# Moving operands of the f32r matmuls placed 192 bytes beyond a multiple of 256 bytes in each partition, their weights on a multiple

## What is computed

```python
# 1: attention, 8 heads of 64, window of n_local = 96 and n_global = 8 first keys
scores = q @ k.T / 8 - slope[h] * dist          # masked where not kept
a = softmax(scores); x = a @ v                  # x: (2, 768, 512)
# 2: gate from a causal convolution of 5 taps over x
gate = sigmoid(conv5(x)); x = (gate * (x @ w_val)) @ w_out1
# 3: the same form with 1024 hidden channels and a centred convolution of 3 taps
h = relu(x @ w_in); y = (h * sigmoid(conv3(h))) @ w_out2
```

## Time and profile before

| | us |
|---|---|
| median of 3 runs | 270.22 (269.54 to 270.37) |
| profiled execution | 269.72 |
| span of its trace | 267.9 |
| PE busy | 261.0 (97%) |
| weight loads (PEld) busy | 205.9 (77%) |
| DVE busy | 190.0 (71%) |
| ACT busy | 151.6 (57%) |
| POOL busy | 47.4 (18%) |

### The profile page before, as it was taken

The page is one execution under the profiler, slowest core; times in us unless marked ns, Lnnn a source line. Parts: engine busy times, 40 slices in busy tenths (PEclk is TensorE's granted clock), DMA queues, the critical chain, the costliest instruction groups (busy, mean ns, idle before and its releaser), DMA issues.

```text
span 267.9 us, 4415 instructions
## 1 busy us (share of the span) xinstructions
PE 261.0 (97%) x1526; PEld 205.9 (77%) x1526; DVE 190.0 (71%) x467; ACT 151.6 (57%) x346; POOL 47.4 (18%) x70
## 2 busy tenths in 40 slices
PE   8899999999999989999999999999999999999995
PEld 7444558788778878888888888888888888888883
DVE  0388479999889977998950897988409998991000
ACT  1051569889998767343554407965537649753100
POOL 1012056695387621200000000000000000000000
PEclk9999999999999999999999999999999999999999
DMA  6999807686897111000000000000000003004021
GB/s 199 355 377 315 289 7 208 203 259 191 240 262 232 45 43 42 4 1 0 2 0 0 0 2 0 1 0 0 2 0 0 0 2 132 24 0 159 0 100 57
DMA packets 20263, 25.16 MB, mean 94 GB/s; under 512 B 3728, under 2 KB 10384, under 8 KB 20112
## 3 DMA queue, kind: packets, MB, share of 16 engines
q1 hardware_dynamic: 19088, 23.86, 27.9%
q10 hardware_dynamic: 1152, 1.01, 1.1%
HBM read 21.52 MB, written 3.34 MB: 93 GB/s over the span
## 4 chain that ended last, share of the span: by engine, by line
PE 85%; DVE 6%; DMA 4%; ACT 3%; issue 1%; ACTq 1%
PE ps L559 21%; PE ps L561 20%; PE ps L560 20%; PE ps L455 8%; PE ps L530 6%; PE ps L515 5%; PE ps L502 5%; DMA win<-in_win 4%; DVE prob L949 2%; ACT prob L699 1%; DVE probT L956 1%; DVE total_eps L960 1%; DVE g L977 1%; DVE xT L972 0%; ACT probT L706 0%
## 5 line engine op out<-in xcount | busy, mean ns | idle before, releaser
L699 ACT ACTIVATE prob<-prob,low 128x256 f32<-128x256 f32 (+1 forms) x96 | 45.9, 482 | 6.6 <-DVE low L949 6.4
L977 DVE SCALAR_TENSOR_TENSOR g<-xT,cw,g 128x512 f32<-128x512 f32 x48 | 34.3, 779 | 1.6 <-ACT g L734 1.6
L805 ACT ACTIVATE h<-ps 128x512 f32<-128x512 f32 x24 | 14.0, 595 | 31.2 <-PE ps L561 31.2
L949 DVE CUSTOM_DVE_ANT_0 prob<-ps,bias 128x256 f32<-128x256 f32 x80 | 30.4, 408 | 1.7 <-PE ps L502 1.7
L455 PE MATMUL ps<-win,w1t 128*128 128x512 f32 x56 | 24.7, 596 | 1.0 <-DMA win<-in_win 1.0
L559 PE MATMUL ps<-gh,Wh 128*128 128x512 f32 x64 | 24.9, 389 | 0.0
L561 PE MATMUL ps<-gh,Wl 128*128 128x512 f32 x64 | 24.9, 389 | 0.0
L561 PE MATMUL ps<-hghA,w2l 128*128 128x512 f32 x64 | 24.9, 389 | 0.0
L560 PE MATMUL ps<-hglA,w2h 128*128 128x512 f32 x64 | 24.9, 389 | 0.0
L559 PE MATMUL ps<-hghA,w2h 128*128 128x512 f32 x64 | 24.9, 389 | 0.0
L560 PE MATMUL ps<-gl,Wh 128*128 128x512 f32 x64 | 24.9, 389 | 0.0
(11 more groups left out here) (101 smaller groups left out, 527.7 us busy)
## 6 DMA issues: line engine op xcount, KB each, us to landing
q_rows<-in_q SPq DMA_DIRECT2D x12, 256.0 KB, 4.8
kW<-in_k SPq DMA_DIRECT2D x12, 256.0 KB, 5.2
v_own<-in_v SPq DMA_DIRECT2D x12, 256.0 KB, 3.3
invT<-inv_turned SPq DMA_DIRECT2D x20, 128.0 KB, 3.4
out<-xT SPq DMA_DIRECT2D x5, 512.0 KB, 2.8
w<-in_w SPq DMA_DIRECT2D x8, 256.0 KB, 11.0
v_win<-in_v SPq DMA_DIRECT2D x10, 192.0 KB, 3.3
prob<-in_wval SPq DMA_DIRECT2D x1, 1024.0 KB, 9.6
```

Source lines behind the costliest of these rows:

```text
L699: act.activation(part, part, ACT.Exp, scale=-1.0, bias=low[:, t % 2, i:i + 1], accum_out=total[:, t % 2, i:i + 1]).then_inc(exp_done, 1)
L805: act.activation(h_cols(m, c), pieces(HB(m), c), ACT.Relu).then_inc(relu_done, 1)
L949: dve.tensor_tensor_reduce(prob[:, t % 2, i, cols], SC(f, e)[:, i % HH // 2, cols], table, -SCALE, 3.0e38, ALU.add, ALU.min, low[:, t % 2, ...
L977: dve.scalar_tensor_tensor(out=pieces(g[:, m, :], c), in0=x_cols(m, c, tap - PAD1), scalar=cw1[:, m, tap:tap + 1], in1=pieces(g[:, m, :], ...
```

## The change

It only moves tensors. Unused tensors of 48 floats (192 bytes) are put ahead of the moving operands' tensors, and fillers behind them bring what follows back to a multiple of 256 bytes. No instruction is added, removed or put elsewhere. The tensors that lie 192 bytes beyond a multiple afterwards are `xh`, `xl`, `gh`, `gl`, `gh_last`, `gl_last`, `hghA`, `hglA`, `hghB`, `hglB`, all moving operands of `product`, and with them the raw `hgA` and `hgB` (read and written by ACT and DVE) and `w2` as it is loaded. `wvh`, `wvl`, `Wh`, `Wl`, `w2h`, `w2l` stay on multiples.

```diff
         over_x = ExitStack()
+        sb("beside_gh_last", [P, 48], where=over_x)
         gh_last, gl_last = sb("gh_last", [P, CT, N], f32r, over_x), sb("gl_last", [P, CT, N], f32r, over_x)
...
         over_W = ExitStack()
+        sb("beside_hghB", [P, 48], where=over_W)
         hghB, hglB = sb("hghB", [P, FT, N], f32r, over_W), sb("hglB", [P, FT, N], f32r, over_W)
         over_W.close()
         raw_over_W = ExitStack()
-        sb("below_hgB", [P, FT, N], where=raw_over_W)
+        sb("below_hgB", [P, FT * N + 48], where=raw_over_W)
         hgB = sb("hgB", [P, FT, N], where=raw_over_W)
         raw_over_W.close()
         Wh, Wl = sb("Wh", [P, CT, F], f32r), sb("Wl", [P, CT, F], f32r)
+        sb("W_to_256_bytes", [P, 64])
...
         over_val = ExitStack()
+        sb("beside_hghA", [P, 48], where=over_val)
         hghA, hglA = sb("hghA", [P, FT, N], f32r, over_val), sb("hglA", [P, FT, N], f32r, over_val)
         over_val.close()
         raw_over_val = ExitStack()
-        sb("below_hgA", [P, FT, N], where=raw_over_val)
+        sb("below_hgA", [P, FT * N + 48], where=raw_over_val)
         hgA = sb("hgA", [P, FT, N], where=raw_over_val)
         raw_over_val.close()
         wvh, wvl = sb("wvh", [P, CT, C], f32r), sb("wvl", [P, CT, C], f32r)
+        sb("beside_xh", [P, 48])
...
         xh, xl = sb("xh", [P, CT, N], f32r), sb("xl", [P, CT, N], f32r)
+        sb("xl_to_256_bytes", [P, 16])
...
         h = sb("h", [P, FT, B * HROW + 1])
-        sb("h_to_256_bytes", [P, 40])
+        sb("beside_gh", [P, 40 + 48])
         gh, gl = sb("gh", [P, CT, N], f32r), sb("gl", [P, CT, N], f32r)
```

## The result

The changed kernel is **slower**: 273.70 us median of 4 runs (272.94 to 274.76) against 269.88 us of the kernel before, 1.015 times, with a 95% interval of 1.012 to 1.019. The forecast was 266.2 us with a range of 261.6 to 271.5, and 0.62 on faster. The time that came is near that of the rival in which the stream doesn't settle, priced at 273.2 us and given a chance of 0.19; it lies beyond the upper end of the range.

The account below looks back on a forecast made before the run. PE was taken to bound the kernel, busy throughout its long f32r stretch at 226.7 ns per matmul. Terms of 0 + 0 - 4.0 us took the median from 270.2 to 266.2 us, range 261.6 to 271.5 us.

Parts of the forecast that it names:

- the stream doesn't settle: Rival: 696 matmuls of the closed stretch keep the start's mean of 231 ns, 3.0 us more, 273.2 us; chance 0.19.
- The covers in front of `hid` and `out`: Remainders are ready before a faster PE needs them; tightest, first half of `gl`, 3.4 us to spare, under 1 us wanted.
- I take half of the best, 5.6 ns, 4.0 us less: Main term, 720 f32r matmul steps on PE: half of the 11.3 ns each, at best 8.1 us, would go.
- the 11.3 ns over the float32 step: Bound on the gain: 226.7 ns less 213.3 + 2.1 ns per f32r matmul, times 720, 8.1 us less.
- the loose steps of the start: First f32r matmuls, between pieces of the attention: 231 ns on the mean, 0.22 to 0.24 us singly; bound on the loss.
- all of the excess goes: Rival: one shift removes the whole 11.3 ns on each of 720 matmuls, 8.1 us less, 262.1 us; chance 0.22.
- a part of the excess going is nearer to the rows than all or nothing: Reason for the main term: a shift changes when the weight and moving streams meet, but hardly keeps them apart; chance 0.40.
- Nothing changes: Rival: the excess belongs to the full rate and the weight change, whatever the addresses; 270.2 us within 0.3%; chance 0.19.

Follow-up runs that it names:

- The map: Matmuls alone, 103 groups, the computation left out: moving operand at every fourth byte from 0 to 252 against weights at 0; 226.7 to 240.1 ns a step.
- 252 bytes: The kernel before with all moving operands 252 bytes beyond a multiple of 256, weights on multiples: 271.41 us, 1.006 times.

## Why the prediction was wrong

**Right.** That PE's step between matmuls is the whole result: 6.67 ns more on each is the loss. That the step depends on how the two streams stand to each other in address; weights moved alone by 64 bytes cost as much as the change. That the excess of 13.4 ns over one cycle per column isn't a price that every change of weights has, since float32 doesn't have it. Which tensors move. That ACT's, DVE's and `w2`'s new places cost nothing. The covers in front of `hid` and `out` weren't tested, since PE didn't get faster.

**Wrong: the step "I take half of the best, 5.6 ns, 4.0 us less".** The term had the right count and the wrong sign: measured +6.67 ns. It took the 11.3 ns over the float32 step as a loss that another address could take away. No address took any of it away: the addresses add 0 to 13.3 ns to it. I had bounded it by the float32 step below and by the loose steps of the start above, and read the bounds as if the value before were a typical place from which any shift could help. The map shows that 226.7 ns is the floor: none of 64 places at 512 columns is below it, eight share it, the middle of the others is 233 ns. From such a start a shift can at best change nothing. The trace had a sign of this that I named and counted for the wrong rival, the one in which all of the excess goes. The stream went through loose steps of 0.22 to 0.24 us and then stayed at 226.7 ns for 623 matmuls without a stray. I argued that a single step of 0.22 us showed that 226.7 wasn't the lowest. But single steps alternate, 225 beside 237 in groups of the map whose mean is 231; only the mean of a rhythm counts, and every mean in these rows was longer than 226.7.

**Wrong: "a part of the excess going is nearer to the rows than all or nothing".** The argument that two streams of different speed must meet, and that a shift moves the meetings, says nothing of the sign. It should have put as much on the slower side as on the faster; instead the range ended at 271.5 us and left most of that side out.

**The rivals.** "All of the excess goes" fails by the same floor. "Nothing changes" fails. Its rule was that of the Trainium skill, page "TensorE: Matmul & The Clock Gate", section "Step-by-step: what each phase is for", that loading weights takes no read bandwidth from the running matmul. Here the place of the weights alone changes the step of f32r by 6.6 ns. So what the prediction drew from the rule, that addresses change nothing, fails for f32r, and the measurement decides; whether it is read bandwidth that the two streams share, no run shows. For bf16 and for float32 the runs agree with the rule, 215.8 and 429 ns at every place tried. "The stream doesn't settle" got the result, 273.2 forecast and 273.7 measured, but not quite the mechanism. The stream does settle, at once, in a rhythm of its own, 231 and 236 ns, and the 231 ns of the loose start that priced it was near by chance: 233.3 is what this place costs, and 68 bytes cost 240.0.

## What to carry to other kernels

For f32r matmuls of 512 columns that each load their weights, keep the moving operands and the weights on a multiple of 256 bytes of a partition, or both 192 bytes beyond one: 226.7 ns a step in this kernel either way. Other distances had 229.0 to 240.0 ns in it, which is 0.6 to 3.3% of its time. The same distance is no guarantee at odd places: 16 against 16 bytes had 230.0 ns. Take the step from starts in the trace, not from a matmul's duration, and when a cost depends on how two streams stand to each other, ask first where in its spread the present value lies. A map of one operation in isolation, 64 places in one run, found that and carried over to 0.1 ns at 0 and 192, and at 68 in one of the two rhythms that this place has; it must read its tiles in the kernel's own order, or it misses what 252 bytes showed.

## What the runs showed of the hardware beyond that

- The mean steps of f32r come in a grid of 3.33 ns: 226.7, 230.0, 233.3, 236.7 and 240.0 ns recur, 8 cycles of the 2.4 GHz clock apart (stretches at a granted clock of 1.00). The single steps repeat in a pattern, 231 and 236 ns for 233.3 in the changed kernel; means between come with patterns of three steps or more (226, 229 and 232 ns at 64 bytes).
- The excess of f32r depends on place and column count together: 11 to 20 ns between 256 and 512 columns at 0 and 192. Place 0, the better of the two at 512 columns, is the worse at 256 and 448.
- With bf16 and plain float32, which take half as many bytes of moving operand per cycle, it is 2 to 3 ns. The floor of 13.3 ns for f32r, why the period is 256 bytes, and why narrow weights don't lower the cost, stay open; no run here tells an access conflict of the two reads from a slot that the next matmul must wait for. The length of the weight load doesn't decide it: at 68 bytes it is 192 ns in the rhythm of 240.0 and 188 in that of 236.7, but in the finer map it is 192 at 200 bytes too, where the step is 233.3, and 188 at 4 bytes, where it is 236.7.
- With moving operands that begin 4 bytes short of a multiple, taking the blocks upwards, each where the one before it ended, costs 3.3 ns a step more on the mean than the same tiles taken downwards.
